# GpSimd's order in the attention steps: values pooled ahead of queries and keys, scatters last

## What is computed

```python
def _attn_ref(q, k, v):                      # 4 batches, 8 heads, 576 positions, head size 64
    factor = 4
    q_d = q.reshape(B, H, Sd, factor, D).mean(axis=3)      # also k_d, v_d: mean of 4 positions
    out_d = sm_attn(q_d, k_d, v_d)                         # softmax attention over 144 positions
    out_up = np.repeat(out_d, factor, axis=2)
    mask = np.abs(pos[:, None] - pos[None, :]) < factor    # band of 7 positions
    ...                                                    # softmax attention inside the band
    return out_up + out_local

def _moe_ref(x, expert_emb, tau, w1, w2):    # 2304 tokens of 512, 8 experts, the best one of each
    ...
        h = np.maximum(x[mask] @ w1[e], 0.0)
        out[mask] = gate_w[mask, None] * (h @ w2[e])

def _moe2_ref(x, w_in, w_out):
    h = x @ w_in
    return np.maximum(0.01 * h, h) @ w_out
```

## Time and profile before

| | |
|---|---|
| time, median of 3 runs | 884.31 us (884.11 to 885.0) |
| time of the profiled execution | 885.43 us |
| its span | 883.7 us |
| TensorE busy (matmul) | 862.7 us (98%) |
| VectorE busy | 537.0 us (61%) |
| ScalarE busy | 506.3 us (57%) |
| GpSimd busy | 204.0 us (23%), nearly all in the first 155 us |
| chain that ended last, by engine | TensorE 81%, GpSimd 9%, "issue" 5%, VectorE 3% |

### The profile page before, as it was taken

The page is one execution under the profiler, slowest core; times in us unless marked ns, Lnnn a source line. Parts: engine busy times, 40 slices in busy tenths (PEclk is TensorE's granted clock), DMA queues, the critical chain, the costliest instruction groups (busy, mean ns, idle before and its releaser), DMA issues.

```text
span 883.7 us, 16199 instructions
## 1 busy us (share of the span) xinstructions
PE 862.7 (98%) x5879; PEld 740.6 (84%) x5879; DVE 537.0 (61%) x782; ACT 506.3 (57%) x910; POOL 204.0 (23%) x279
## 2 busy tenths in 40 slices
PE   8999979999999999999999999999999999999997
PEld 5887868788888888888888998998998998998996
DVE  6776776899999999999986543233223223224222
ACT  5777677888889888898885443222223223223222
POOL 8766675451010032520000002002002002001000
PEclk9998999999999999999999999999999999999999
DMA  8686476448577376621001002002002001000000
GB/s 243 197 230 204 137 229 249 170 153 295 206 257 286 100 293 175 179 81 45 31 25 47 1 1 72 1 1 71 0 0 71 0 0 59 13 0 36 2 0 36
DMA packets 44866, 92.66 MB, mean 105 GB/s; under 512 B 4616, under 2 KB 23928, under 8 KB 40704
## 3 DMA queue, kind: packets, MB, share of 16 engines
q1 hardware_dynamic: 34752, 43.95, 16.5%
q0 software_dynamic: 9872, 47.53, 15.2%
q10 hardware_dynamic: 176, 0.31, 0.1%
HBM read 72.97 MB, written 18.81 MB: 104 GB/s over the span
## 4 chain that ended last, share of the span: by engine, by line
PE 81%; POOL 9%; issue 5%; DVE 3%; ACT 1%; DMA 0%; DVEq 0%; POOLq 0%; SPq 0%; ACTq 0%
PE banks L1039 74%; PE banks L1101 2%; POOL pin L586 2%; POOL vpool L594 1%; POOL vpool L595 1%; PE banks L1046 1%; POOL pool_a L577 1%; POOL pool_a L574 1%; PE banks L1020 1%; POOL xs L612 1%; PE banks L1121 1%; DVE elo L1758 1%; POOL kd L578 1%; POOL qd L575 1%; PE banks L815 1%
## 5 line engine op out<-in xcount | busy, mean ns | idle before, releaser
L1758 DVE TENSOR_TENSOR elo<-wslot,ehi 128x1024 fp32r<-128x1024 f32 x196 | 237.0, 1226 | 19.2 <-ACT ehi L1349 13.0
L1349 ACT ACTIVATE ehi<-wslot 128x1024 fp32r (+1 forms) x196 | 205.8, 1059 | 19.2 <-PE banks L1039 18.1
L1852 DVE SCALAR_TENSOR_TENSOR fg<-fraw 128x384 f32<-128x384 f32 x96 | 53.5, 557 | 212.3 <-ACT fraw L1467 200.1
L1467 ACT ACTIVATE fraw<-banks 128x384 f32<-128x384 f32 x96 | 47.2, 492 | 228.2 <-PE banks L1039 224.5
L1039 PE MATMUL banks<-zhi,winhi 128*128 (+1 forms) x384 | 130.5, 340 | 0.2 <-DVE winlo L1776 0.2
L1039 PE MATMUL banks<-zhi,winlo 128*128 (+1 forms) x384 | 129.4, 337 | 0.0
L1039 PE MATMUL banks<-zlo,winhi 128*128 (+1 forms) x384 | 128.9, 336 | 0.0
L1039 PE MATMUL banks<-wouthi,fhi 128*128 128x512 f32 x288 | 113.1, 393 | 2.9 <-DVE flo L1857 2.5
L1039 PE MATMUL banks<-wouthi,flo 128*128 128x512 f32 x288 | 113.9, 395 | 0.0
L1039 PE MATMUL banks<-woutlo,fhi 128*128 128x512 f32 x288 | 113.7, 395 | 0.0
L799 POOL DMA_INDIRECT out_x<-o_sb,row_tok x15 | 15.0, 1000 | 318.8 <-ACT o_sb L1494 315.8
(11 more groups left out here) (233 smaller groups left out, 1461.4 us busy)
## 6 DMA issues: line engine op xcount, KB each, us to landing
wslot<-in_w POOLq DMA_DIRECT2D x24, 1024.0 KB, 7.0
wslot<-in_w SPq DMA_DIRECT2D x8, 1024.0 KB, 6.2
xr<-xs SPq DMA_DIRECT2D x25, 272.0 KB, 2.8
ys<-y_sb SPq DMA_DIRECT2D x25, 256.0 KB
qb<-in_qT SPq DMA_DIRECT2D x16, 288.0 KB, 4.2
vq<-in_vtok SPq DMA_DIRECT2D x32, 144.0 KB
kb<-in_kT SPq DMA_DIRECT2D x15, 288.0 KB, 5.6
vwin<-in_vtok SPq DMA_DIRECT2D x16, 245.0 KB
```

Source lines behind the costliest of these rows:

```text
L1349: act.activation(ehi[:, ring_at(k), :], wslot[:, chunk_cols(offs[dt], matrix, half, c)], ACT.Copy).then_inc(s_ehi, 1)
L1467: act.activation(fraw[:, f % 2, :], banks[:, f % 2, 0:TB], ACT.Copy).then_inc(s_fhev, 1)
L1758: dve.tensor_tensor(elo[:, ring_at(k), :], wslot[:, chunk_cols(offs[dt], matrix, half, c)], ehi[:, ring_at(k), :].bitcast(F32), ALU.subtra ...
L1852: dve.scalar_tensor_tensor(out=fg[:, f % 2, :], in0=fraw[:, f % 2, :], scalar=0.01, in1=fraw[:, f % 2, :], op0=ALU.mult, op1=ALU.max).then ...
```

## The change

GpSimd's steps are put in another order; no instruction is added or removed on any engine. From step 8 on, `pool_v(s-1)` stands right behind `normalise(s-1)`, ahead of `pool_qk(s+2)`; below step 8 it stays behind `pool_qk`. The scatter of a step comes last in it. The scatter of step 16 (tile 3 of batch 1) leaves the loop and comes behind `indices(B - 2)`, and waits for the outputs of pair 14 instead of pair 13. The constants of `slot_no` and `indices(B - 2)` are written into step 16, where they stand behind the same `pool_v(15)` as before.

```diff
--- before.py
+++ after.py
@@ -387,7 +387,7 @@
             return x[:, :, 0], x[:, :, 1]
 
         N2 = TILES[B - 2][1] - TILES[B - 2][0]
-        SCATTER_AT = {9: (0, 0), 10: (0, 1), 11: (0, 2), 12: (0, 3), 13: (1, 0), 14: (1, 1), 15: (1, 2), 16: (1, 3)}
+        SCATTER_AT = {9: (0, 0), 10: (0, 1), 11: (0, 2), 12: (0, 3), 13: (1, 0), 14: (1, 1), 15: (1, 2)}
         QUARTER_AT = (4, 7, 10, 13)
         DRAIN = NPAIR - LAG
 
@@ -646,24 +646,29 @@
                     gp.dma_start(xs[DUMMY:DUMMY + P, :], zrow[:]).then_inc(s_zrow, 16)
                 if 2 <= s <= NPAIR:
                     normalise(s - 1)
+                if s >= 8 and 0 <= s - 1 < NPAIR:
+                    pool_v(s - 1)
                 if s + 2 < NPAIR:
                     pool_qk(s + 2)
                 if s == 0:
                     constants_as_floats()
                 if s == 1:
                     normalise(s - 1)
+                if 0 <= s - 1 and s < 8:
+                    pool_v(s - 1)
+                if s == NPAIR:
+                    gp.wait_ge(s_score, 2 * NPAIR)
+                    link(gp.iota(slot_no_i[:], pattern=[[1, P]], base=0, channel_multiplier=0))
+                    gp.tensor_copy(slot_no[:], slot_no_i[:]).then_inc(s_slot_no, 1)
+                    indices(B - 2)
                 if s in SCATTER_AT:
                     b, k = SCATTER_AT[s]
                     if k == 0:
                         indices(b)
                     gp.wait_ge(s_o6, s - 2)
                     scatter(b, k, 1)
-                if 0 <= s - 1 < NPAIR:
-                    pool_v(s - 1)
-            gp.wait_ge(s_score, 2 * NPAIR)
-            link(gp.iota(slot_no_i[:], pattern=[[1, P]], base=0, channel_multiplier=0))
-            gp.tensor_copy(slot_no[:], slot_no_i[:]).then_inc(s_slot_no, 1)
-            indices(B - 2)
+            gp.wait_ge(s_o6, NPAIR - 1)
+            scatter(1, 3, 1)
             gp.wait_ge(s_t2, NPAIR)
             scatter(1, 4, 1)
             gp.wait_ge(s_o6, NPAIR)
```

## The result

The changed kernel takes 875.55 us (median of 4 runs, 875.42 to 875.78) where the kernel before, on the same chip, takes 884.65 us (4 runs, 884.11 to 887.9). The ratio is 0.989, with a 95% interval of 0.9866 to 0.9914: 9.1 us faster, where 10.3 were forecast. The profiled execution took 875.68 us, its span was 873.9 us.

What follows compares the result with a forecast made beforehand. It took a ring of waits between GpSimd and VectorE, 8.8 us a step, to hold up TensorE's 7.21. A gain of 12.2 less 1.4, 10.8 us, gave 874.6 or 873.5, stated as 874.0 us; range 871.5 to 880.

Steps and rivals of the forecast that it cites:

- The ring: Steps with a scatter: GpSimd and VectorE wait for each other, 7.00 + 1.8 = 8.8 us a step, holding up TensorE.
- Values and queries/keys: GpSimd's steps: values end about 2.8 us in instead of 7.0 to 7.65; queries and keys 1.42 us later, costing nothing.
- margins of 0 to 1.4 us: TensorE's needs in its steps: probabilities, scores' inputs and `add_down` rows all arrive in time, by 0 to 1.4 us.
- The 12.2 us less 1.4: Step 16's token counting begins 12.2 us earlier; 1.4 taken off for margins that will not all hold, leaving 10.8 us.
- The sum: TensorE's work at full clock from 79.56 us on, without stopping, reaches step 16's token counting at 119.3 instead of 131.51.
- The moved scatter: Drain: its 1.01 us fall into GpSimd's 3.84 us wait and cost nothing, or 1.3 us if too late.
- VectorE blocked by GpSimd: Rival, in the steps: shared ports make reciprocals 1.63 us later each step; gain 8.5, time 876 us; chance 0.15.
- Half clock: Rival: TensorE falls to 1.2 GHz once, in the drain or early experts; gain 7.4, time 877 us; chance 0.10.
- The handover: Rival, start of the experts: weight transfers come no earlier and eat the gain, 884 us; chance 0.08, other waits included.
- TensorE at 1.2 GHz for good: Rival: short waits in each step keep TensorE at the low clock; 25 us lost against 10.8, 899 us; chance 0.05.

Runs made afterwards that it cites:

- e1: The kernel before, with only the scatter moved behind the values, queries and keys staying ahead of them: 874.28 us, ratio 0.986.
- e4: The kernel before, GpSimd's order untouched, with VectorE doing `add_v` behind the reciprocals instead of ahead of them: 879.59 us, ratio 0.9929.
- e8: The kernel before, with the first pooling of the queries done twice in steps 9 to 13: 889.42 us against 889.96, ratio 1.0022.
- e7: The changed kernel, with step 15's scatter also in the drain and queries and keys ahead of the values in all steps: 873.71 us, ratio 0.9879.
- e3: The changed kernel, but the scatter of step 16 stays behind the normalising of pair 15, as before: 874.04 us, ratio 0.9877.
- e2: The changed kernel, but in steps 9 to 15 the scatter stands between the values and queries and keys: 875.78 us, ratio 0.9876.
- second profile: Profiled execution of a repeat run of the unedited changed kernel; the repeat's median was 873.77 us, ratio 0.9868.
- c_before_again: The kernel before, unedited, run once more for a second profile: 884.23 us.
- c_after_again: The changed kernel, unedited, run once more: 873.77 us, ratio 0.9868.

## Why the prediction came out right

**The ring.** Right, and shown from three sides: with the scatter taken out of it, it is no longer than TensorE's step (`e1`); cut on VectorE, it leaves GpSimd's steps to follow one another without a wait (`e4`); and 0.74 us more in it lengthen each step by 0.65 to 0.74 (`e8`). GpSimd's steps were forecast at 78.9, 85.9, 93.1, 100.1, 107.8 and 113.4 and came at 79.56, 86.56, 94.40, 101.34, 108.82 and 114.68. With the 0.70 us by which step 9 began late here (71.91 against the 71.21 that the sum started from), the first two are right to 0.1 us. From step 12 on they are a further 0.3 to 0.6 us late, as TensorE's scores are (86.00, 93.55, 100.75 and 107.97 for 84.8, 92.3, 99.5 and 106.7).

**What freed it.** Here the prediction credited more than was needed. It followed the values to 2.8 us into the step and did not ask whether 5.4 would have done. `e1` shows that it does: a ring of 7.2 us is no longer than TensorE's step. Of the three edits, the scatter's place has all of the gain, the values' place ahead of queries and keys adds none that can be measured (873.77 against `e1`'s 874.28, measured at another time, and 873.71 for `e7`), and the scatter of step 16 adds none (`e3`).

**Values and queries/keys.** Right. Nobody waits for values that come early, and queries and keys cost nothing where they are 1.42 us later; they cost 1.7 us in all where they are about a scatter later (`e2`), so the margins of 0 to 1.4 us were sized about right.

**The 12.2 us less 1.4.** TensorE reached the counting of step 16 43.34 us behind the scores of step 11. The sum had 41.74 without losses (119.3 - 77.56) and 43.1 with them. The losses have rows: 0.49 us for `x_sb` and 0.48 for `ohb` above, 0.43 once in the scores of step 11, and 0.1 to 0.2 in small gaps. The second profile, without the 0.43, has 42.83. The size is right, though the reason given for it (margins that don't hold) covers at most the 0.48, so luck had a part in it. The 0.49 was no lost margin: the kernel before has the same wait in step 16 (at 124.19), and the sum passed over it.

**The moved scatter.** In its new place it starts at 126.11 us, behind 2.71 us of idleness:

```profile
126.11 1.43 POOL L612 DMA_INDIRECT xs<-x_sb,pidx  x1 [2.71 <-PE banks L940]
```

The prediction put it into a wait at that place, at a price of nothing; it holds.

**VectorE blocked by GpSimd.** Real: `vd` took 0.84, 0.83 and 0.67 us in three steps and `cand` 1.80 once. The Trainium skill (SBUF — State Buffer, Who interferes with whom) counts an addition with two inputs in SBUF among those that meet GpSimd's reads; these rows agree. But in the changed kernel they fall into VectorE's slack, except for the last, which leaves 0.48 us for TensorE. The rival's price of 3.7 us (12.2 - 8.5) was too high here: it charged 1.63 us to each step. In the order of `e4` the same blocking does cost time (`vd` of up to 2.19 us, above): there the values are released right ahead of the normalising, here ahead of short poolings.

**Half clock.** It did not come between 0 and 150 us of the first profile of the changed kernel, nor behind 80 us of its second. **The handover** ate nothing: 752.2 us behind the counting, before and after. **TensorE at 1.2 GHz for good** did not happen.

**Against the median.** 874.0 was forecast; 875.55 and, at another time, 873.77 were measured. The difference between these two is not in the change. The kernel before isn't fixed either: the sum was taken from an execution with 1.16 us of half clock in its steps, and from `c_before_again`, with 52.30 us for the stretch, the same 41.74 and 1.4 would have given 9.2 us instead of 10.8. Measured were 9.1 and, at the other time, 10.8. The first profile has 0.80 us at its start, 0.43 in the scores of step 11 and 0.27 in the drain, which I can place but not explain.

## What to carry to other kernels

When two engines wait for each other by turns, write the ring down as a length: the work from one's release to its result, plus the other's answer. Compare it with the step of the engine that should be the bound; whatever is on one engine's list and not in the ring's result (here a scatter) goes behind that result. Once the ring was no longer than the bound's step, more reordering bought nothing here, and the list's own length was the next limit: 7.00 against 7.21 us, so that one more instruction of 0.7 us in five steps cost 2.9.

## What the runs showed of the hardware

**A VectorE addition can be held by a scatter, and by two GpSimd instructions in a row.** `cand`, 128x32 with both inputs in SBUF, began 0.84 us into the scatter's 1.18 and ended at 120.20, just behind the end of the next normalising at 118.78 + 1.36 = 120.14: 1.80 us for 0.19, and 1.79 or 1.80 in `c_after_again`, `e1`, `e2` and `e3`. In the kernel before the same addition was held by a scatter alone:

```profile
128.85 1.01 POOL L612 DMA_INDIRECT xs<-x_sb,pidx  x1 [0.16 <-issue]
...
129.52 0.42 DVE L1615 TENSOR_TENSOR cand<-L_all,lmax 128x32 f32<-128x32 f32 x1
```

It ended at 129.94, 0.08 us behind the scatter. Not every scatter does that: in the drain of the changed kernel `cand` began 0.94 us into one (132.62 + 0.97) and took 0.20 us (at 133.56). What decides it no run here shows. Nor does it take a scatter for a hold over two instructions: the `vd` of 2.19 us in `e4` began with the normalising and ended 0.29 us behind the pooling after it (94.14 + 0.66).

**The same idleness does not always bring the half clock.** TensorE's wait of 1.84 us in step 11 came ahead of a clock of 0.56 in one execution of the kernel before and left it at 1.00 in `c_before_again`. The wait of 2.08 us in step 15, the longest, did the opposite: `c_before_again` has 0.50 behind it (above), the first execution 1.00:

```profile
114.28:124.19 9.91, 7.34 (x136) 6.20 (x135) 7.50 (x17) 7.30 (x22) 6.08 (x8) 1.00 0.45 147
```

The low clock lasted about 11 us in the first (0.50 still from 91 to 92 us, 1.00 from 93 on) and 3.4 us in the other. The Trainium skill (TensorE: Matmul & The Clock Gate, Part 1) calls the warm-up run-variable; these two lengths agree, and the rows show the same for the fall.

**Starts differ from execution to execution.** `c_after_again`'s profiled execution took 876.83 us, 3.06 above its median, and has a clock of 0.61 between 20 and 24 us (above); it reached step 11 3.0 us late (80.70, where `e7` did at 77.67). The one of `e4` had 0.55 between 20 and 39 us and reached the scores of step 6 at 48.68, where the kernel before did at 41.23. These two starts came 3.0 and 7.4 us late, which is of the size by which the runs of one kernel spread; that such starts make up the whole spread is not shown. They are why stretches of the traces were compared here.
